# Rests of w_out's pieces and of the attention tiles' x on VectorE, and the first tile's products spread chunk by chunk

## What is computed

```python
k_p = k.reshape(B, H, Sp, 8, D).mean(axis=3)      # v_p likewise, Sp = 72
attn = softmax(q @ k_p.T / sqrt(D)); x = attn @ v_p
x = x.transpose(0, 2, 1, 3).reshape(4608, 512)
h = x @ w1_in;  g = maximum(0.01 * h, h);         x = g @ w1_out
h = x @ w2_in;  g = h * clip(h + 3, 0, 6) / 6;    out = g @ w2_out
```

## Time and profile before

| | us |
|---|---|
| median of 3 runs | 1787.67 (1785.9 to 1789.25) |
| the profiled execution, its own time | 1780.07 |
| its span, first to last instruction | 1778.3 |
| TensorE busy | 1708.0 (96%) |
| VectorE busy | 1018.2 (57%) |
| ScalarE busy | 640.8 (36%) |
| GpSimd busy | 650.6 (37%) |
| granted TensorE clock, mean | 0.987 |

### The profile page before, as it was taken

The page is one execution under the profiler, slowest core; times in us unless marked ns, Lnnn a source line. Parts: engine busy times, 40 slices in busy tenths (PEclk is TensorE's granted clock), DMA queues, the critical chain, the costliest instruction groups (busy, mean ns, idle before and its releaser), DMA issues. The chain is left out here.

```text
span 1778.3 us, 34260 instructions
## 1 busy us (share of the span) xinstructions
PE 1708.0 (96%) x10794; PEld 1508.7 (85%) x10794; DVE 1018.2 (57%) x1786; ACT 640.8 (36%) x1305; POOL 650.6 (37%) x716
## 2 busy tenths in 40 slices
PE   7888999999999999999999999999999999999999
PEld 7676878887888878888999788889898989898898
DVE  8664775757667576765454555444445454545444
ACT  4443333333333332333232334343334343333333
POOL 6657867535444443543251523030303030211200
PEclk8899999999999999999999999999999999999999
DMA  5734567767768676675978766666767576767662
GB/s 143 238 124 158 185 227 249 251 209 219 232 197 259 193 235 214 197 241 166 309 231 290 232 211 195 201 204 188 222 176 220 172 223 174 221 171 219 176 199 79
DMA packets 218113, 366.83 MB, mean 206 GB/s; under 512 B 22464, under 2 KB 47040, under 8 KB 218048
## 3 DMA queue, kind: packets, MB, share of 16 engines
q1 hardware_dynamic: 218048, 366.04, 66.1%
HBM read 308.28 MB, written 57.67 MB: 206 GB/s over the span
## 5 line engine op out<-in xcount | busy, mean ns | idle before, releaser
L1372 PE MATMUL ps_h<-xs_hi,ring 128*128 128x256 f32 x3808 | 819.2, 283 | 25.7 <-issue 8.5
L1372 PEld LDWEIGHTS ps_h<-xs_hi,ring 128*128 128x128 f32 x3808 | 642.0, 188 | 75.8 <-issue 37.3
L1372 PE MATMUL ps_h<-xs_lo,ring 128*128 128x256 f32 x1904 | 533.7, 280 | 0.0
L1372 PEld LDWEIGHTS ps_h<-xs_lo,ring 128*128 128x128 f32 x1904 | 359.6, 189 | 28.1
L946 ACT ACTIVATE g_hi<-gate 128x512 fp32r<-128x512 f32 x288 | 181.9, 632 | 426.1 <-DVE gate L1132 238.3
L1165 DVE TENSOR_TENSOR u<-ps_h,p 128x256 f32<-128x256 f32 x272 | 114.6, 421 | 208.7 <-PE ps_h L1372 182.4
L1324 PE MATMUL ps_y<-g_hi,wout_hi 128*128 128x512 f32 x576 | 229.3, 398 | 0.2
L1326 PE MATMUL ps_y<-g_hi,wout_lo 128*128 128x512 f32 x576 | 228.6, 397 | 0.0
L1324 PE MATMUL ps_y<-wout_hi,g_hi 128*128 128x512 f32 x576 | 226.2, 393 | 1.4 <-DVE y_stage L1161 1.4
L1326 PE MATMUL ps_y<-wout_hi,g_lo 128*128 128x512 f32 x576 | 226.9, 394 | 0.0
L1325 PE MATMUL ps_y<-g_lo,wout_hi 128*128 128x512 f32 x576 | 226.7, 394 | 0.0
(11 more groups left out here) (126 smaller groups left out, 2362.4 us busy)
## 6 DMA issues: line engine op xcount, KB each, us to landing
ring<-w_in_split SPq DMA_DIRECT2D x920, 256.0 KB, 2.8
w_in_split<-ring SPq DMA_DIRECT2D x56, 256.0 KB, 3.8
w_in_split<-stage SPq DMA_DIRECT2D x56, 256.0 KB, 4.2
k_raw<-in_kT SPq DMA_DIRECT2D x32, 288.0 KB, 3.6
q_raw<-in_qT SPq DMA_DIRECT2D x32, 288.0 KB, 4.1
v_raw<-in_v SPq DMA_DIRECT2D x32, 288.0 KB
x0T<-x_stage SPq DMA_DIRECT2D x32, 288.0 KB, 3.9
x1T<-y_stage SPq DMA_DIRECT2D x36, 256.0 KB, 3.9
```

What stands on the lines that cost most here:

```text
L1372: mm = pe.matmul(banks[BANK_OF[r]], a, b[:, r, c, :], start=r in OPENS and c == 0 and n == 0, stop=c == 1 and n == 2, skip_group_check=True)
```

## The change

- `piece_lo` moves from GpSimd to VectorE for all 16 pieces: the first layer's in steps 0 to 5 of tile 0 (FIRST_PIECE_AT), the second's at the ends of step 7 of tile 8 and of steps 1, 3 and 5 of tile 9 (LATE_PIECE_AT).
- `x_lo` for tiles 1 to 7 moves to VectorE, one rest at a time, in the last step of the tile before and the first places of the tile itself (X_LO_AT, FIRST_X_LO_AT; an entry of 8 or more is in the next tile). GpSimd keeps their t sums, and both parts for tiles 8 to 17.
- ACT rounds the x of tiles 1 to 7 later (X_HI_AT, FIRST_X_HI_AT), for the others in the order it had (LATE_X_HI_AT).
- In tile 0 a chunk of the plain product is issued at a time, over places up to 5, with the groups of the second product between them; the copies of h, the gate and its rest move with them.
- Tile 0 has its own tables for attention and its DMAs (FIRST_UNIT_PLACES, FIRST_LOAD_PLACES and so on).
- GpSimd's `blocks_lo(3)` comes in front of `sum_v(1, 1)`.

```diff
+FIRST_UNIT_PLACES = [(0, 6, 7, 9, 10, 13, 15, 16, 18),
+                     (14, 19, 20, 21, 22, 24, 26, 27, 29),
+                     (25, 30, 31, 32, 33, 35, 37, 38, 40),
+                     (36, 41, 42, 43, 44, 46, 48, 49, 51)]
+FIRST_LOAD_PLACES = (4, 18, 29, 40)
+FIRST_STORE_PLACES = (20, 31, 42, 52)
+FIRST_X_PLACES = (22, 33, 44, 54)
+FIRST_X_HI_AT = (3, 5, 5, 6, 6, 7, 7)
+FIRST_X_LO_AT = (4, 6, 6, 7, 7, 8, 9)
+X_HI_AT = (2, 4, 4, 5, 5, 6, 7)
+X_LO_AT = (3, 5, 5, 6, 7, 8, 9)
+LATE_X_HI_AT = (0, 1, 2, 3, 4, 5, 7)
+LATE_PIECE_AT = ((7, 6), (7, 7), (1, 6), (1, 7), (3, 6), (3, 7), (5, 6), (5, 7))
+FIRST_PIECE_AT = ((0, 7), (1, 0), (2, 0), (2, 1), (4, 0), (4, 1), (5, 0), (5, 1))
...
@@ gpsimd
-            piece_lo(0)
-            piece_lo(1)
             sum_k(1, 1, 16)
             blocks_lo(2)
+            blocks_lo(3)
             sum_v(1, 1, 18)
...
             t_sums(1)
             sums_lo(0)
-            x_lo(1)
             first_sums(1)
...
                 stores2_done(i + 1)
-                split_x(T + 1)
+                t_sums(T + 1)
...
@@ scalar, first_step
-                    if m == 0:
+                    if m == 2:
                         act.wait_ge(first_done, 2 * i + 1)
...
-                    if m == 2:
+                    if m == 5:
                         act.wait_ge(first_done, 2 * i + 2)
...
-                    if m == 3:
+                    if m == 4:
                         g_hi_of(i, i, 1, 0)
...
@@ vector
+            def piece_lo(piece):
+                _, raw_w, hi, lo = piece_views(piece)
+                dve.wait_ge(w_hi_ready, piece + 1)
+                nc.vector.tensor_tensor(lo, raw_w, hi.bitcast(F32), ALU.subtract
+                                        ).then_inc(w_ready, 1)
+            def x_lo(T, r):
+                dve.wait_ge(x_hi_ready, PRODUCTS * (T - 1) + r + 1)
+                nc.vector.tensor_tensor(xs_lo[:, r], x_block(r), xs_hi[:, r].bitcast(F32),
+                                        ALU.subtract).then_inc(x_ready, 1)
...
                 for m in range(HF):
+                    if (i, m) in FIRST_PIECE_AT:
+                        piece_lo(FIRST_PIECE_AT.index((i, m)))
                     attention_at(0, HF * i + m)
-                    if m == 1:
+                    if m == 3:
                         gate_of(i, 1, 0)
-                    if m == 3:
+                    if m == 5:
                         g_lo_of(i, i, 1, 0)
+                    next_x(0, i, m)
...
@@ tensor, first_step
                 first_part(i, 1, 0)
+                first_part(i, 1, 1)
                 lagging(2, 0, 2)
                 place(0)
-                first_part(i, 1, 1)
+                first_part(i, 1, 2)
                 lagging(2, 0, 3)
                 place(1)
-                first_part(i, 0, 0)
+                first_part(i, 1, 3)
                 lagging(1, 1, 0)
                 place(2)
+                first_part(i, 0, 0)
                 first_part(i, 0, 1)
                 lagging(1, 1, 1)
                 place(3)
+                first_part(i, 0, 2)
                 lagging(1, 1, 2)
                 place(4)
+                first_part(i, 0, 3)
                 lagging(1, 1, 3)
                 place(5)
```

## The result

The changed kernel takes 1761.23 us, median of 3 runs (1760.43 to 1762.57), against 1787.67. The ratio is 0.9853, 95% interval 0.9831 to 0.9876: 26.4 us faster, where 37 were predicted. The time lies inside the range of 1741 to 1770, but outside the forecast's own 1743 to 1757, and all five terms of the sum came out smaller than they were priced, the first one by only 0.7 us, and one of them has the wrong sign.

What follows compares the result with a forecast made beforehand. TensorE, busy for 96% of the span, was taken as the bound, with only idle and slow stretches to win. Terms 15.0 + 7.9 + 4.8 + 4.1 + 5.5 = 37.3 us off 1787.7 gave 1751 us, range 1741 to 1770.

Steps and rivals of the forecast that it cites:

- tile 0: First tile: 15.0 us of stalls and 5.0 of slow clock go, 5 stay or are new; gain 15.0 us.
- A: VectorE's new rests, in tile 0 and at seven tile starts, wait for GpSimd: 1768 us, chance 0.15.
- B: Tile 0's queues: SP or GpSimd stand behind blocks_lo(3), two of four stalls stay or return: 1760 us, chance 0.2.
- The price of a piece's rest on VectorE: Tile 0: a 128x1024 subtraction on VectorE was taken at 1.2 us, within bounds of 1.2 and 2.4.
- the rule against the sum: Moved rests: two-input VectorE instructions contend with GpSimd ones reading SBUF; whoever issues first blocks the other entirely. No size given.
- Rival D: Tile 0's stalls come from the schedule's ends, not the port, and the other gains fail too: 1787 us, chance 0.04.
- The start of tile 1: TensorE's 6.11 us wait and slow clock behind it shrink to 1.5 us left; gain 7.9 us.
- The start of tile 2: The 2.82 us wait for an x rest and 3.1 us by the clock shrink to 1.1; gain 4.8 us.
- Tiles 3 to 6: Four waits of 1.13 us for the keys' rest at the tile starts go; gain 4.1 us, including 0.3 at tile 7.
- The cover is the idle time at the end of step 7: Starts of tiles 3 to 6: 1.4 us idle, plus time won on q and k rests, covers VectorE's x rests.
- C: Tile starts: VectorE becomes the bound at seven starts, slower from a 2.8 us wait each: 1803 us, chance 0.03.
- Tile 9: Second layer's first tile: of 7.0 us too much, 1.5 stay once VectorE makes the pieces' rests; gain 5.5 us.

Runs made afterwards that it cites:

- e6: The kernel before with only the rests of the 16 pieces moved to VectorE, at the changed kernel's places: 1772.63 us, ratio 0.9928.
- e8: The kernel before with only the spread products and the first tile's own tables, all rests on GpSimd: 1772.63 us, ratio 0.9932.
- e12: The changed kernel with GpSimd's v sum of unit (2, 0) moved behind the first block sum's rests: 1756.85 us, ratio 0.984.
- e2: The changed kernel with VectorE's loop over tiles 2 to 6 written out: 1749.38 us, ratio 0.9805.
- e3: The changed kernel with roundings and rests of pieces 8 and 9 one step earlier, in step 6 of tile 8: 1755.9 us, ratio 0.9837.

## Why the prediction was right or wrong, point by point

*The direction: right; the range: right with some luck.* The direction came by tile 0, which gave 14.3 us in the profiled runs against the 15.0 of the sum. But the traces show 19.6 of the 37.3 us that were added up, and 1761 lies in the part of the range that was there for rivals A and B, of which neither came as described. A further 6.8 us of the 26.4 are there because the old kernel's profiled execution lay 7.6 below its median and the new one's 0.8; the prediction took its gain, read from that fast execution, off the median. Its stalls that are left:

```profile
70.78 0.69 PE L1456 MATMUL ps_att<-ident,prob 96*72 96x96 f32 x6 [0.89 <-DVE prob L1248]
74.43 0.40 PE L1360 MATMUL ps_att<-pT_hi,v_hi 72*128 72x288 f32 x1 [1.53 <-DVE pT_lo L1253]
114.75 0.69 PE L1456 MATMUL ps_att<-ident,prob 96*72 96x96 f32 x6 [0.90 <-DVE prob L1248]
74.40:80.00 5.60, 5.57 (x24) 4.65 (x25) 4.14 (x7) 3.85 (x8) 0.00 (x0) 0.70 0.68 198
```

The third pair's probabilities are 0.90 late, as worked out (0.9); the first pair's 0.89 (0.5), and its pv0 1.53 (0.4). TensorE's idle time in the tile is 3.6 us in all, inside the 3 to 5 of the sum. One stretch of slow clock behind a stall, 5.6 us at 0.70, is left, 1.7 us; as much again is lost in the tile's first 3.4 us, at 0.51, a stretch that comes from the prologue and that the sum did not look at. The two tests "no stall above 1.5 us" and "clock 0.98" were missed by 0.03 us and by 0.01. Passed were the gates (none above 1.22 us), the length (106.9) and the first product of tile 1, right behind the last of tile 0; that one says little, since the second product waits.

*The price of a piece's rest on VectorE: right in the median.* Assumed 1.2 us, the mean is 1.41; over the 16 of them (columns: ns least, median, most):

```profile
L1159 DVE TENSOR_TENSOR wout_lo<-wout_raw,wout_hi x16: 1157/1221/2321, 62.7 to 1053.0; 128x1024 fp32r<-128x1024 f32 x16
```

*What made tile 0 slow: half right.* The reading put the late probabilities to GpSimd's subtractions. The fills without reads and the pieces alone show that contention and schedule both had a share, 3.3 and 2.4 us of the first stall. The sum held because the change treats both. Of the rule against the sum, the rows bear out one half, that the two engines contend; the other, that whoever issues first blocks the other, they do not: the gate began at 115.84, GpSimd's pair at 116.35, and the gate still ended behind both the earlier trace rows. Rival D, that it was all schedule, falls with `e6`, which keeps the old schedule and wins 8.1 us there; that the schedule has a share is shown by `e8`, which wins 11.2 with GpSimd's subtractions in place. Rival B, stalls that stay in tile 0's queues, did not come: no store of x0 stands behind a long wait there.

*The start of tile 1: mis-sized, 7.9 against 2.7.* Left were to be 1.5 us; there are 3.4 us of waits in the rows shown and 5.0 x 0.32 = 1.6 by the clock. The step that failed is "at the starts of tiles 1 to 6 GpSimd has just ended t_sums, so a moved rest meets little". At tile 1 the x rests run beside the t sums, and both lengthen. These 5.0 us leave a gain of 4.4, and 2.7 were measured; where the rest went stays open. TensorE's idle time over the tile fell only from 12.4 to 10.2 us. `e12` confirms GpSimd's part and shows VectorE behind it. A second trace of the changed kernel had 118.4 us for this tile, so the gain varies from nothing to 2.7.

*The start of tile 2: mis-sized, 4.8 against 2.9.* Left were to be 1.1 us; the wait for an x rest shrank from 2.82 to 1.28, the slow clock went, and a wait for h is new. The step that failed is the same as at tile 1: x rests took 1.17 and 1.72 us there, where 0.69 was counted.

```profile
277.31 0.38 PE L1407 MATMUL ps_h<-xs_hi,ring 128*128 128x256 f32 x1 [1.28 <-DVE xs_lo L1165]
282.90 0.35 PE L1407 MATMUL ps_h<-xs_hi,ring 128*128 128x256 f32 x1 [1.12 <-ACT h L1059]
```

*Tiles 3 to 6: wrong sign, +3.8 against -3.4.* The wait for the keys' rest went as said, and VectorE's q rest fell from 1.82 us to 0.75. The step that failed is "The cover is the idle time at the end of step 7, 1.4 us", with the 1.0 us won on the q rest. The rests did fit in it, since `e2` shows u before TensorE needs it. But the loop's jump stands behind them, and it had become one with a fetch, 2.1 us in the open; the sum put it at nothing, and I had not asked what more instructions do to a loop. Without it the term is positive, and larger than priced: with the loop written out the four tiles take 424.0 us, 7.0 less than before. By the other traces (above) the loss with the jump is nearer 2 than 3.4.

*Rivals A and C: their sign without their cause.* Waits for u at every start of tiles 3 to 6 were to speak for A or C. They came, by the jump. Single rests do take 1.7 to 1.9 us beside GpSimd (tiles 1 and 2) and a pair of pieces 4.55 (tile 9), so A's mechanism exists at three places, and mildly in tile 0, where two of the eight pieces took 1.5 and 1.8; not at seven starts and eight pieces. C was to turn the result at a wait of 2.8 us for each start; 0.45 + 1.27 + 1.15 = 2.87 are reached in the rows of tile 3. What saved the result is C's other half: the 3 us by the clock were not paid, the clock being granted at 1.00 there:

```profile
384.00:394.00 10.00, 7.14 (x50) 5.60 (x49) 6.82 (x14) 3.39 (x9) 0.00 (x0) 1.00 0.61 168
```

*Tile 9: mis-sized, 5.5 against 3.8.* Left were to be 1.5 us; the waits are 1.05 and 0.65, and the tile still takes 2.8 more than the next one (84.6). The pieces were priced alone, with GpSimd at work beside them at this one place; `e3` takes both waits away by moving them. The test "86 us" for this tile was missed by 1.4.

## What to carry to other kernels

When rests or copies move to a less loaded engine, look at each new place for what the other engine does at that moment: the same subtraction took 0.69 us alone and 1.9 beside a sum on GpSimd, and both were slower. Before instructions are added to a loop, count the instruction queue's packets for one turn of it: a body that ran without a fetch can begin to fetch, and the jump back cost 2 us here that no busy time shows, only a gap put down to "issue". And two cures of one stall need not add: measure each alone and on top of the other before their gains are summed, with enough runs to tell a difference of 2 us, which these did not.

## What the runs showed of the hardware

- The jump back of VectorE's loop took 3.1 to 3.2 us at all four turns of the changed kernel and left gaps of 1.99 to 2.14 us, with a fetch of 8 KB of instructions inside each gap; in the kernel before the jump took 0.2 to 0.3 us, there were no fetches at the jumps looked at, and writing the loop out changed nothing.
- GpSimd's fills of 128x1024 (0.96 us) let VectorE's gate and its rests run at 0.68 to 0.69 us, while a pair of its subtractions of the same size held a gate for 6.56 us. A small operation with one input (96x12, 0.17 us where GpSimd is idle) was held to the end of GpSimd's instruction by both: 0.93 us beside a fill, 2.33 beside a subtraction.
- A 128x1024 rest takes 1.22 us on VectorE and 2.41 on GpSimd.
- Behind the three waits at the start of tile 3 the clock stayed at 1.00, that is 2.4 GHz; behind the waits at the start of tile 1 it was granted at 0.68 for 5 us, partly 1.2 GHz. The 3 us by the clock that rival C added to every wait are paid at some waits only.
